# A routed two-mixture kernel: the second mixture's router logits from VectorE instead of TensorE, indices from VectorE, two result banks, scatter two steps behind, a packed schedule

## The chip, the cores and the metric

The kernel runs on one core of a Trainium2 chip. The metric is the device time of one execution in microseconds (us). The kernel before takes 753.04 us, the median of three runs (751.76 to 753.70).

## The reference

Attention over chunks of 64 tokens, then two mixtures of 8 experts (D = 512, F = 1024) over the same N = 2304 tokens; the second has a capacity of 576 tokens for an expert.

```python
x = attention_by_chunks(q, k, v)                  # 2304 x 512
# mixture 1 (w1, w2, w_gate, w_output_gate)
logits = x @ w_gate;  e = argmax(logits)
g = softmax(logits)[e] * sigmoid((x @ w_output_gate)[e])
x = g * (relu(x @ w1[e]) @ w2[e])
# mixture 2 (w1, w2, w_gate, capacity)
logits = x @ w_gate;  e = argmax(logits)          # these logits are what the change moves
g = softmax(logits)[e], 0 for tokens past an expert's capacity
out = g * (relu(x @ w1[e]) @ w2[e])
```

## The kernel before

**Stages.** Attention over 18 tiles of 128 tokens; routing 1; mixture 1 (in the code m = 0); routing 2; mixture 2 (m = 1). Routing sorts tokens by expert and pads each expert to whole tiles of 128: 20 tiles in either mixture. By the inputs, the tiles of experts 0 to 7 are 4, 1, 4, 3, 2, 1, 3, 2 in mixture 1 and 4, 4, 2, 5, 1, 2, 1, 1 in mixture 2.

**A tile.** POOL gathers 128 rows of x by an indirect DMA (`xg`). TensorE transposes them (L993), VectorE splits them in a high and a low part (`x_split`, L812 and L814), and TensorE forms the first product of 24 matmuls of 512 columns (three for each pair of chunk and half: high by high weights, low by high, high by low; L998 to L1000). VectorE applies relu (L804), TensorE transposes the hidden rows (L1020), VectorE splits them (`hidden_high` L821, `hidden_low` L827), and the second product, again 24 matmuls, goes to one PSUM bank. VectorE multiplies it by the gate (`scaled`, L842) into `y`, and POOL scatters `y` by an indirect DMA (L528). In mixture 1 the second mixture's router logits are formed beside it: TensorE transposes `y` (`result_T`, L1039), VectorE copies (`y_copy`, L835), TensorE multiplies by `wgate2` (`result_logits`, L1045), VectorE copies 8 columns behind the 512 of `y` (`logits_copy`, L846), and the scattered row has 520 columns.

**Order.** Each engine runs a written-out loop over tiles. `step(g)` on TensorE: transposes of h(g), first product of g+1, transposes of x(g+2), second product of g; in mixture 1 the transposes and the logits of y(g-1) lie inside the first product of g+1. `step(g)` on VectorE follows it, `scaled(g)` last. `scaled(g)` waits until scatter g-1 has landed, since there is one `y`, and the second product of g waits for `scaled(g-1)`, since there is one result bank.

**Weights.** An expert has 8 pieces of 512 KB (4 of w1, 4 of w2). SyncE loads a piece into one of 4 ring buffers, ScalarE rounds it to `wh` (L607), POOL subtracts to `wl` (`low_parts`, L423) and thereby frees the ring buffer. `wh` and `wl` hold two experts, so ScalarE waits for the last tile of the expert two before. A table made in routing (`pieces`, `middles`) tells POOL how many pieces to do in each of its steps. POOL's `step(g)`: read three entries of the table, pieces, scatter g-1, gather g+3, pieces. Before the scatter and before the gather POOL copies an index column (`sidx` L522, `gidx` L511) and waits for its own copy.

**Routing 2.** While VectorE works on the tables, POOL issues gather 0, does four pieces (the second half of expert 1's), and issues gather 1. `link` puts a wait between each VectorE instruction of the routing and the next.

Of the kernel before, what the change touches and what calls it, by code (L numbers as in the profile page):

```python
# [13 lines left out]
P = 128  # L14
# [9 lines left out]
def build(nc, q, k, v, wg1, wog1, w1a, w2a, wg2, w1b, w2b, cap, out):  # L24
# [31 lines left out]
    with ctx:  # L56
# [32 lines left out]
        wgate2 = sb("wgate2", [P, DC, E])  # L89
# [28 lines left out]
        scatter_at = [sb(f"scatter_at{m}", [P, NTAB], I32) for m in range(2)]  # L118
# [3 lines left out]
        pieces = [sb(f"pieces{m}", [P, NTAB], I32) for m in range(2)]  # L122

        middles = [sb(f"middles{m}", [P, NTAB], I32) for m in range(2)]
# [22 lines left out]
        at_pos = sb("at_pos", [P, 2, P, NH2], BF16)  # L147
        in_tile = sb("in_tile", [P, 2, NTAB, NH2], BF16)
        at_tile = sb("at_tile", [P, 2, NV, NTAB, NH2], BF16)
        at_gate = sb("at_gate", [P, 2, NG, NTAB, NH2], BF16)  # L150
        xg = sb("xg", [P, ROW])
        yT = sb("yT", [P, DC, P])
        h = sb("h", [P, F])
# [12 lines left out]
        hTh = sb("hTh", [P, FC, P], F32R)  # L166
        hTl = sb("hTl", [P, FC, P], F32R)
# [13 lines left out]
        ps_h, ps_hT, ps_y, ps_yT, ps_xT = b01, b23, b45[:, 0:BANK], b45[:, BANK:2 * BANK], b6  # L181
        ps_rank, ps_slot, ps_gate = b6, b7, b45

# [3 lines left out]
        s_w = sem("s_w")  # L187
        s_zero = sem("s_zero")
# [60 lines left out]
        yT_done = sem("yT_done")  # L249
        yT_here = sem("yT_here")  # L250
        yl_done = sem("yl_done")
        yl_here = sem("yl_here")
        si_here = [sem(f"si_here{m}") for m in range(2)]
# [5 lines left out]
        def at(x, g):  # L259

            return x[:, g:g + 1] if isinstance(g, int) else x[:, bass.ds(g, 1)]

# [132 lines left out]
        def _(pool):  # L395
# [35 lines left out]
            def due(m, g):  # L431


                lo = pool.value_load(at(pieces[m], g)[0:1, :], min_val=PX, max_val=2 * E * PX)
                hi = pool.value_load(at(pieces[m], g + 1)[0:1, :], min_val=PX, max_val=2 * E * PX)
                middle = pool.value_load(at(middles[m], g)[0:1, :], min_val=PX, max_val=2 * E * PX)
                return lo, middle, hi
# [14 lines left out]
            for m in range(2):  # L452
# [53 lines left out]
                def gather(g):  # L506

                    if reached(g, 1):
                        pool.wait_ge(g_in[m], g * 16)
                        pool.wait_ge(xT_done[m], g)  # L510
                    nc.gpsimd.tensor_copy(gidx[:, :], at(gather_at[m], g)).then_inc(gi_here[m], 1)  # L511
# [6 lines left out]
                def scatter(g):  # L518

                    if reached(g, 1):  # L520
                        pool.wait_ge(y_out[m], g * 16)
# [3 lines left out]
                    if m == 0:  # L525
                        pool.wait_ge(yl_here, g + 1)
# [5 lines left out]
                def step(g, ahead=True):  # L532
# [4 lines left out]
                    if reached(g, 1):  # L537
                        scatter(g - 1)
# [3 lines left out]

                step(0)
                with pool.Fori(1, total - 2) as g:
                    step(g)
                step(total - 2, ahead=False)
                step(total - 1, ahead=False)
                scatter(total - 1)
# [5 lines left out]
        def _(act):  # L554
            act.dma_start(wgate1[:, :, 0:E], wg1.rearrange("(c p) e -> p c e", p=P)).then_inc(s_w, 16)
            act.dma_start(wgate1[:, :, E:2 * E], wog1.rearrange("(c p) e -> p c e", p=P)).then_inc(s_w, 16)
            act.dma_start(wgate2[:, :, :], wg2.rearrange("(c p) e -> p c e", p=P)).then_inc(s_w, 16)
# [61 lines left out]
            act.wait_ge(routed, 1)  # L619
# [15 lines left out]
        def _(dve):  # L635
# [65 lines left out]
            for m in range(2):  # L701
# [129 lines left out]
                def y_copy(j):  # L831
                    dve.wait_ge(yT_done, j + 1)
                    if reached(j, 1):
                        dve.wait_ge(yl_done, j)
# [267 lines left out]
```

## Time and profile before

| what | us |
|---|---|
| median of three runs | 753.04 |
| the profiled execution's own time | 754.11 |
| its span, first to last instruction | 752.4 |
| mean granted TensorE clock (share of full) | 0.929 |
| TensorE busy | 642.0 (85%) |
| VectorE busy | 356.8 (47%) |
| POOL busy | 419.8 (56%) |
| ScalarE busy | 180.3 (24%) |

Attention takes the span to about 108 us, routing 1 to 124, mixture 1 to 430, routing 2 to 459, mixture 2 to the end. A group of the page gives the source line, the engine, the operation, the tiles that it writes and reads, the busy time and the idle time before it with what ended that. The rows that count stand in the section after the change.

### The profile page before, as it was taken

Reading aid. Unit: us, or ns where it says so; the run is one execution under the profiler, and the core shown is the slowest. Engines: PE = TensorE matmul, PEld = TensorE weight load, DVE = VectorE, ACT = ScalarE, POOL = GpSimd, SP = SyncE. Lnnn points to the kernel's source line nnn. Section 1 sums busy time; section 2 is a strip of 40 time slices with the busy share of each in tenths; the row PEclk is TensorE's granted clock in tenths of the full one; section 3 lists DMA queues with packets and bytes.
Section 4 is the critical chain, followed back from the end, with each engine's and each line's share of the span. In section 5 each row is a group of like instructions: output and inputs, shape, how many; then the busy total and the mean of one; then the engine's idle time right before and its main releaser. Section 6 shows DMA issues by size and latency. Waiting matters only on the chain.

```text
span 752.4 us, 15054 instructions
## 1 busy us (share of the span) xinstructions
PE 642.0 (85%) x4310; PEld 529.1 (70%) x4311; DVE 356.8 (47%) x652; ACT 180.3 (24%) x223; POOL 419.8 (56%) x351
## 2 busy tenths in 40 slices
PE   4898855999999999999987534999999999998653
PEld 3787844788887888877876423788888878886542
DVE  3887745454354354354334084545454364433240
ACT  2577631002420112422322200022023200243200
POOL 1046442256685657779778342116657763579760
PEclk9999985999999999999998655999999999999796
DMA  9999993043444425445554313114325532355500
GB/s 198 233 297 283 271 337 125 29 140 137 157 156 152 154 79 174 175 154 186 178 176 155 110 37 104 44 34 153 126 87 177 182 126 84 112 174 195 191 32 21
DMA packets 79690, 111.64 MB, mean 148 GB/s; under 512 B 28249, under 2 KB 46681, under 8 KB 79664
## 3 DMA queue, kind: packets, MB, share of 16 engines
q1 hardware_dynamic: 67616, 86.00, 37.0%
q0 software_dynamic: 8000, 25.17, 9.9%
q10 hardware_dynamic: 4048, 0.12, 0.3%
q8 instruction: 17, 0.28, 0.2%
q14 instruction: 9, 0.07, 0.0%
HBM read 92.48 MB, written 20.00 MB: 150 GB/s over the span
## 4 chain that ended last, share of the span: by engine, by line
PE 50%; POOL 14%; issue 12%; DVE 10%; POOLq 5%; DMA 5%; ACT 1%; ACTq 1%; DVEq 0%; SPq 0%
PE b L998 12%; PE b L999 12%; POOL wl L423 12%; PE b L1000 12%; PE b L925 2%; PE b L1020 2%; PE b L993 2%; PE b L903 2%; DVE owner L773 1%; DVE kT L665 1%; POOLq L423 1%; PE b L1045 1%; DVE xrow L676 1%; DMA x<-y,sidx 1%; PE b L913 1%
## 5 line engine op out<-in xcount | busy, mean ns | idle before, releaser
L423 POOL TENSOR_TENSOR wl<-ring,wh (+1 forms) x128 | 302.0, 2386 | 43.0 <-issue 21.3
L607 ACT CAST wh<-ring 128x1024 f32 (+1 forms) x112 | 112.8, 1047 | 479.2 <-PE b L1000 387.3
L998 PE MATMUL b<-wh,xTh 128*128 x320 | 135.0, 422 | 5.7 <-DVE xTl L814 3.7
L998 PE MATMUL b<-wh,hTh 128*128 x320 | 132.5, 414 | 7.5 <-DVE hTl L827 7.5
L842 DVE TENSOR_SCALAR y<-b,gates 128x512 f32<-128x512 f32 x40 | 30.0, 751 | 227.0 <-PE b L1000 103.2
L999 PE MATMUL b<-wh,xTl 128*128 x320 | 129.0, 403 | 0.0
L999 PE MATMUL b<-wh,hTl 128*128 x320 | 128.9, 403 | 0.0
L1000 PE MATMUL b<-wl,xTh 128*128 x320 | 128.0, 400 | 0.0
L1000 PE MATMUL b<-wl,hTh 128*128 x320 | 127.9, 400 | 0.0
L804 DVE TENSOR_SCALAR h<-b 128x512 f32<-128x512 f32 x80 | 54.8, 689 | 78.3 <-PE b L1000 78.1
L998 PEld LDWEIGHTS b<-wh,hTh 128*128 128x128 f32 x320 | 61.8, 193 | 21.3 <-issue 7.7
L998 PEld LDWEIGHTS b<-wh,xTh 128*128 128x128 f32 x320 | 61.6, 193 | 19.1 <-issue 7.2
L1000 PEld LDWEIGHTS b<-wl,hTh 128*128 128x128 f32 x320 | 61.3, 192 | 15.1
L1000 PEld LDWEIGHTS b<-wl,xTh 128*128 128x128 f32 x320 | 61.3, 192 | 14.8
L999 PEld LDWEIGHTS b<-wh,hTl 128*128 128x128 f32 x320 | 61.8, 193 | 12.8
L999 PEld LDWEIGHTS b<-wh,xTl 128*128 128x128 f32 x320 | 61.8, 193 | 11.4
L514 POOL DMA_INDIRECT xg<-x,gidx x36 | 37.8, 1049 | 31.4 <-POOL gidx L511 30.5
L827 DVE TENSOR_TENSOR hTl<-b,hTh 128x512 fp32r<-128x512 f32 x80 | 52.7, 680 | 0.0
L821 DVE CAST hTh<-b 128x512 fp32r<-128x512 f32 x80 | 51.1, 681 | 0.0
L993 PE MATMUL b<-ident,xg 128*128 128x128 f32 x168 | 26.8, 284 | 25.2 <-DMA xg<-x,gidx 12.2
L427 POOL DMA_DIRECT2D x<-xrow x18 | 10.2, 566 | 63.3 <-DVE xrow L676 63.3
L993 PEld LDWEIGHTS b<-ident,xg 128*128 128x128 f32 x168 | 21.5, 147 | 32.3 <-DMA xg<-x,gidx 13.5
(142 smaller groups left out, 663.1 us busy)
## 6 DMA issues: line engine op xcount, KB each, us to landing
ring<-in_moe_w SPq DMA_DIRECT2D x128, 512.0 KB, 3.2
vin<-in_v SPq DMA_DIRECT2D x72, 64.0 KB, 4.9
x<-xrow POOLq DMA_DIRECT2D x18, 256.0 KB, 6.1
out<-zeros SPq DMA_DIRECT2D x18, 256.0 KB, 3.8
qin<-in_q SPq DMA_DIRECT2D x6, 512.0 KB, 7.5
kin<-in_k SPq DMA_DIRECT2D x6, 512.0 KB, 6.9
qin<-in_q SPq DMA_DIRECT2D x2, 384.0 KB, 5.6
kin<-in_k SPq DMA_DIRECT2D x2, 384.0 KB, 5.9
```

The lines of the kernel that those rows point to most:

```text
L423: nc.gpsimd.tensor_tensor(low, src, high.bitcast(F32), ALU.subtract).then_inc(wl_here, 1)
L514: nc.gpsimd.indirect_dma_start(xg[:, 0:src.shape[1]], None, src, bass.IndirectOffsetOnAxis(ap=gidx[:, 0:1], axis=0), bounds_check=N - 1, o ...
L607: nc.scalar.copy(dst, ring[:, i % RING]).then_inc(wh_here, 1)
L804: nc.vector.tensor_scalar_max(h[:, cols], ps_h[:, cols], 0.0).then_inc((h0_here, h1_here)[half][m], 1)
L821: nc.vector.tensor_copy(hTh[:, chunks, :], ps_hT[:, half * BANK:(half + 1) * BANK].rearrange("p (c t) -> p c t", t=P)).then_inc((hTh0_here ...
L827: nc.vector.tensor_tensor(hTl[:, chunks, :], ps_hT[:, half * BANK:(half + 1) * BANK].rearrange("p (c t) -> p c t", t=P), hTh[:, chunks, :] ...
L842: nc.vector.tensor_scalar(y[:, 0:D], ps_y, at(gates[m], j), None, ALU.mult).then_inc(y_here[m], 1)
L903: last = nc.tensor.transpose(ps_aT[:, c * P:(c + 1) * P], xrow[:, (t - 1) % XS, c].rearrange("p e d -> p (e d)"), ident[:, :])
L993: last = nc.tensor.transpose(ps_xT[:, c * P:(c + 1) * P], xg[:, c * P:(c + 1) * P], ident[:, :])
L998: nc.tensor.matmul(dst, high, weights(wh, *wt), start=start, stop=False)
L999: nc.tensor.matmul(dst, low, weights(wh, *wt), start=False, stop=False)
L1000: return nc.tensor.matmul(dst, high, weights(wl, *wt), start=False, stop=stop)
```

## The change

- The logits of mixture 2: `wg2_rows` holds the router's 8 columns, each as a row of 512 on every partition (2 MB by one broadcast DMA on ScalarE's queue, behind routing 1). For every tile and expert VectorE issues one `scalar_tensor_tensor` of 128x512 (result x gate x row, with the sum as the accumulator's output): 8 a tile, of tile g-1 in step g, four behind relu(g+1, 0) and four behind `x_split(g+2)`. The transposes of y, both copies and the product with `wgate2` go.
- Two result banks take turns (`result_bank`); in mixture 1 `scaled(g-1)` stands at the end of step g, and the scatter is two steps behind.
- `gidx` and `sidx` are written by VectorE, out of PSUM copies of the tables (`next_rows`, and in `scaled`); POOL's two copies go.
- The schedule is one integer for a step, taken apart in registers, instead of three entries.
- The four pieces that POOL did inside routing 2 become part of mixture 2's schedule.
- The load of `wgate2` at the start goes.

```diff
@@ POOL
-                lo = pool.value_load(at(pieces[m], g)[0:1, :], ...)
-                hi = pool.value_load(at(pieces[m], g + 1)[0:1, :], ...)
-                middle = pool.value_load(at(middles[m], g)[0:1, :], ...)
+                cuts = pool.value_load(at(schedule[m], g)[0:1, :], min_val=0, max_val=2 ** 24 - 1)
+                lo, middle, hi = pool.snap(cuts % 256), pool.snap(cuts // 256 % 256), pool.snap(cuts // 65536)
...
                 if m == 1:
-                    for i in range((E + 1) * PX + PW, (E + 2) * PX):
-                        low_parts(i, i % RING)
                     pool.wait_ge(s_zero, 16 * NT)
...
-                    nc.gpsimd.tensor_copy(gidx[:, :], at(gather_at[m], g)).then_inc(gi_here[m], 1)
                     pool.wait_ge(gi_here[m], g - 2)
...
-                    nc.gpsimd.tensor_copy(sidx[:, :], at(scatter_at[m], g)).then_inc(si_here[m], 1)
-                    pool.wait_ge(si_here[m], g + 1)
-                    pool.wait_ge(y_here[m], g + 1)
+                    pool.wait_ge(y_here[m], g + 2)
...
-                        scatter(g - 1)
+                        scatter(g - behind)          # behind = (2, 1)[m]
@@ VectorE, routing
-                done = FIRST if m == 0 else (E + 2) * PX
+                done = FIRST if m == 0 else (E + 1) * PX + PW
...
+                # two more linked instructions pack pieces and middles into schedule[m],
+                # one more writes ps_gather; scatter_at becomes ps_scatter (PSUM)
@@ VectorE, mixtures
+                def next_rows(g):
+                    dve.wait_ge(xT_done[m], g)
+                    nc.vector.tensor_copy(gidx[:, :], at(ps_gather, g)).then_inc(gi_here[m], 1)
...
                 def scaled(j):
                     dve.wait_ge(y_done[m], j + 1)
                     if reached(j, 1):
                         dve.wait_ge(y_out[m], j * 16)
-                    nc.vector.tensor_scalar(y[:, 0:D], ps_y, at(gates[m], j), None, ALU.mult).then_inc(y_here[m], 1)
+                    nc.vector.tensor_copy(sidx[:, :], at(ps_scatter, j))
+                    if m == 0:
+                        dve.wait_ge(next_lg_here, (j + 1) * E)
+                        nc.vector.tensor_copy(y[:, D:ROW], next_lg)
+                    nc.vector.tensor_scalar(y[:, 0:D], result_bank(dve, j), at(gates[m], j), None,
+                                            ALU.mult).then_inc(y_here[m], 1)
+
+                def next_logits(j, experts):
+                    dve.wait_ge(y_done[m], j + 1)
+                    dve.wait_ge(y_here[m], j + 1)
+                    for e in experts:
+                        if e >= 2:
+                            dve.wait_ge(next_lg_here, j * E + e - 1)
+                        nc.vector.scalar_tensor_tensor(
+                            out=unread[:, e % 2], in0=result_bank(dve, j), scalar=at(gates[m], j), in1=wg2_rows[:, e, :],
+                            op0=ALU.mult, op1=ALU.mult, accum_out=next_lg[:, e:e + 1]).then_inc(next_lg_here, 1)
@@ TensorE
-                def result_T(j): ...          # 4 transposes of y
-                def result_logits(j): ...     # 4 products with wgate2
                 def second_product(g, first, before):
+                    dst = result_bank(pe, g)
```

VectorE's loop over the tiles of mixture 1, before (`hTh`, `hTl` are the hidden rows' parts, `xTh`, `xTl` those of x, b is any PSUM bank):

```order
L821 CAST hTh<-b 128x512 x2
L827 TENSOR_TENSOR hTl<-b,hTh 128x512
L834 REGISTER_ALU
L835 COPY yT<-b 128x512
L827 TENSOR_TENSOR hTl<-b,hTh 128x512
L800 REGISTER_ALU
L804 TENSOR_SCALAR h<-b 128x512
L846 COPY y<-b 128x8
L804 TENSOR_SCALAR h<-b 128x512
```

The same place now (`unread` is the product that nobody reads, `wg_rows` the router's rows):

```order
L837 CAST hTh<-b 128x512 x2
L843 TENSOR_TENSOR hTl<-b,hTh 128x512 x2
L811 REGISTER_ALU
L815 TENSOR_SCALAR h<-b 128x512
L866 ISA
L866 REGISTER_ALU
L866 SCALAR_TENSOR_TENSOR unread,b<-b,gates,wg_rows 128x512 x2
L865 ISA
L866 SCALAR_TENSOR_TENSOR unread,b<-b,gates,wg_rows 128x512
L865 REGISTER_ALU
L866 SCALAR_TENSOR_TENSOR unread,b<-b,gates,wg_rows 128x512
L815 TENSOR_SCALAR h<-b 128x512
```

The copy of the transposed y is gone and four multiply-and-sums stand between the two relus; four more stand at the end of the loop.

POOL in routing 2, before (`part` is the gate's last part of the routing):

```order
L481 TENSOR_TENSOR part<-rest,part 128x18
L488 DMA xg<-x,gather_at 128x520
L423 TENSOR_TENSOR wl<-ring,wh 128x1024 x4
L488 DMA xg<-x,gather_at 128x520
L270 TENSOR_LOAD ends
```

And now:

```order
L489 TENSOR_TENSOR part<-rest,part 128x18
L496 DMA xg<-x,gather_at 128x520 x2
L279 TENSOR_LOAD ends
L279 ISA x2
L496 DMA xg<-x,gather_at 128x520
```

The four pieces between gather 0 and gather 1 are gone from this place.

POOL's loop over the tiles of mixture 1, scatter and gather, before:

```order
L521 ISA
L522 ISA
L522 COPY sidx<-scatter_at 128x1
L528 DMA x<-y,sidx 2304x520
L509 ISA
L511 ISA
L511 COPY gidx<-gather_at 128x1
L514 DMA xg<-x,gidx 128x512
```

And now:

```order
L448 UNCONDITIONAL_BRANCH
L524 DMA x<-y,sidx 2304x520
L514 REGISTER_ALU
L516 DMA xg<-x,gidx 128x512
L448 REGISTER_ALU
```

Both copies are gone, and the two indirect DMAs stand one behind the other.

## Rows read from the trace of the kernel before

**Rows 1.** Page, part 4: the chain that ended last, by engine and line

```profile
PE b L998 12%; PE b L999 12%; POOL wl L423 12%; PE b L1000 12%; PE b L925 2%; PE b L1020 2%; PE b L993 2%; PE b L903 2%; DVE owner L773 1%; DVE kT L665 1%; POOLq L423 1%; PE b L1045 1%; DVE xrow L676 1%; DMA x<-y,sidx 1%; PE b L913 1%
```

**Rows 2.** Windows: one step of mixture 1 or 2 each; busy us (instructions)

```profile
core 0: us, PE busy (x) PEld busy (x) DVE busy (x) ACT busy (x) POOL busy (x), PEclk, DMA share, GB/s
136.03:149.82 13.79, 12.90 (x62) 10.24 (x61) 6.80 (x11) 0.00 (x0) 3.92 (x4) 1.00 0.11 39
163.67:177.51 13.84, 13.84 (x73) 11.52 (x72) 6.67 (x11) 3.89 (x4) 3.77 (x5) 1.00 0.11 39
497.14:509.65 12.51, 12.51 (x62) 10.23 (x60) 5.82 (x9) 3.89 (x4) 3.61 (x4) 1.00 0.13 42
```

**Rows 3.** Timeline of TensorE: steps 0 and 19 of either mixture start

```profile
136.03 0.60 PE L1020 MATMUL b<-ident,h 128*128 128x128 f32 x4
...
406.46 1.03 PE L1020 MATMUL b<-ident,h 128*128 128x128 f32 x8
...
470.83 1.17 PE L1020 MATMUL b<-ident,h 128*128 128x128 f32 x8
...
724.92 1.03 PE L1020 MATMUL b<-ident,h 128*128 128x128 f32 x8
```

**Rows 4.** Waits: us in total, times, longest

```profile
DVE y L842 <- DMA x<-y,sidx: 59.9, 10, 6.7
...
DVE iota_f L638 <- DMA cap_i<-in_capacity: 8.7, 1, 8.7
PE b L1039 <- DVE y L842: 9.6, 8, 2.7
```

**Rows 5.** Timeline of VectorE in mixture 1: start, us, what

```profile
207.09 0.75 DVE L842 TENSOR_SCALAR y<-b,gates 128x512 f32<-128x512 f32 x1 [5.70 <-DMA x<-y,sidx]
207.75 1.28 DVE L821 CAST hTh<-b 128x512 fp32r<-128x512 f32 x2
...
214.37 0.68 DVE L812 CAST xTh<-b 128x512 fp32r<-128x512 f32 x1
215.09 0.69 DVE L814 TENSOR_TENSOR xTl<-b,xTh 128x512 fp32r<-128x512 f32 x1
```

**Rows 6.** Timeline of VectorE: small and SBUF-to-SBUF instructions, attention and routing 2

```profile
9.71 0.17 DVE L642 CAST values<-token_i 128x36 bf16<-128x36 int32 x1
9.80 0.14 DVE L643 CAST cap_f<-cap_i 128x1 f32<-128x1 int32 x1
...
433.82 0.33 DVE L712 SCALAR_TENSOR_TENSOR order<-chosen,expert_no 128x144 f32<-128x144 f32 x1
...
437.65 0.31 DVE L735 TENSOR_TENSOR chosen<-chosen,over 128x144 f32<-128x144 f32 x1
```

**Rows 7.** Timeline of VectorE: the owner table in routing 1 and in routing 2

```profile
120.30 0.18 DVE L773 TENSOR_SCALAR owner<-owner_f 128x28 int32<-128x28 f32 x1
...
445.69 10.02 DVE L773 TENSOR_SCALAR owner<-owner_f 128x28 int32<-128x28 f32 x1
455.75 0.19 DVE L774 TENSOR_TENSOR soon<-owner_f 128x25 f32<-128x25 f32 x1
```

**Rows 8.** Timeline of POOL, routing 2 and the end of mixture 1

```profile
427.34 0.98 POOL L528 DMA_INDIRECT x<-y,sidx  x1 [4.77 <-DVE y L846]
...
446.42 9.24 POOL L423 TENSOR_TENSOR wl<-ring,wh 128x1024 fp32r<-128x1024 f32 x4
```

**Rows 9.** Timeline of POOL near the end of mixture 2

```profile
677.25 18.82 POOL L423 TENSOR_TENSOR wl<-ring,wh  x8
696.02 0.18 POOL L522 COPY sidx<-scatter_at 128x1 int32 x1
697.16 1.03 POOL L528 DMA_INDIRECT out<-y,sidx  x1 [0.96 <-POOL sidx L522]
698.19 0.20 POOL L511 COPY gidx<-gather_at 128x1 int32 x1
699.29 1.05 POOL L514 DMA_INDIRECT xg<-x,gidx  x1 [0.90 <-POOL gidx L511]
702.05 2.36 POOL L423 TENSOR_TENSOR wl<-ring,wh  x1 [1.72 <-issue]
```

**Rows 10.** Timeline, same stretch: TensorE, then VectorE's last waits

```profile
702.77 1.11 PE L993 MATMUL b<-ident,xg 128*128 128x128 f32 x4 [9.40 <-DMA xg<-x,gidx]
...
730.59 0.75 DVE L842 TENSOR_SCALAR y<-b,gates 128x512 f32<-128x512 f32 x1 [9.22 <-DMA out<-y,sidx]
```

More of the change, by code:

```diff
@@ L146, in build, with routed_by @@
             xrow = early("xrow", [P, XS, G, 2, DH])
[L147 to L150, printed above, removed]
+        with ExitStack() as routing:
+            def routed_by(name, shape):
+                return routing.enter_context(nc.sbuf_tensor(name, shape, BF16))
+            at_pos = routed_by("at_pos", [P, 2, P, NH2])
+            in_tile = routed_by("in_tile", [P, 2, NTAB, NH2])
+            at_tile = routed_by("at_tile", [P, 2, NV, NTAB, NH2])
+            at_gate = routed_by("at_gate", [P, 2, NG, NTAB, NH2])
+        hTh = sb("hTh", [P, FC, P], F32R)
+        hTl = sb("hTl", [P, FC, P], F32R)
+        h = sb("h", [P, F])
         xg = sb("xg", [P, ROW])
-        yT = sb("yT", [P, DC, P])
-        h = sb("h", [P, F])
         y = sb("y", [P, ROW])
@@ L165, in build @@
         xTl = sb("xTl", [P, DC, P], F32R)
[L166 to L167 removed]
+        unread = sb("unread", [P, 2, D])
+        wg2_rows = sb("wg2_rows", [P, E, D])
         b01 = bank("b01", 2)
@@ L541, in step @@
                     split(middle, hi)
+                behind = (2, 1)[m]
                 step(0)
-                with pool.Fori(1, total - 2) as g:
+                if m == 0:
+                    step(1)
+                    step(2)
+                with pool.Fori((3, 1)[m], total - 2) as g:
                     step(g)
@@ L547, in _ @@
                 step(total - 1, ahead=False)
+                if m == 0:
+                    scatter(total - 2)
                 scatter(total - 1)
@@ L619, in _ @@
             act.wait_ge(routed, 1)
+            for u in range(XS):
+                act.wait_ge(x_out[u], 16 * (NT // XS))
+            act.dma_start(wg2_rows[:, :, :].rearrange("p e d -> p (e d)"),
+                          wg2.rearrange("e d -> (e d)").unsqueeze(0).partition_broadcast(P)).then_inc(wg2_in, 16)
             with act.Fori(2, E) as e:
@@ L865, in step @@
                     if m == 0 and reached(g, 1):
-                        logits_copy(g - 1)
+                        next_logits(g - 1, range(0, E // 2))
                     if not tail:
                         relu(g + 1, 1)
+                        next_rows(g + 3)
                         x_split(g + 2)
-                    scaled(g)
+                    if m == 0 and reached(g, 1):
+                        next_logits(g - 1, range(E // 2, E))
+                        scaled(g - 1)
+                    if m == 0 and not reached(g, 1):
+                        dve.wait_ge(wg2_in, 16)
                     if m == 0 and tail:
-                        y_copy(g)
-                        logits_copy(g)
+                        next_logits(g, range(E))
+                    if m == 1 or tail:
+                        scaled(g)
                 expert_steps(dve, m, step)
@@ L1029, in second_product @@
                         for c in range(half * FC // 2, (half + 1) * FC // 2):
[L1030 removed]
+                            last = product(dst, hTh[:, c, :], hTl[:, c, :], (first, D * F // P // BANK + c),
                                            start=(c == 0), stop=(c == FC - 1))
                     last.then_inc(y_done[m], 1)
[L1034 to L1047 removed]
                 def step(g, head=False, tail=False):
```

97 lines of the change are left out of this document (30 added, 67 removed).

## The prediction

> **What bounds the kernel now.** I read the chain first [rows 1]: TensorE's product lines L998 to L1000 hold 36% of the span and POOL's low parts 12%, and a single VectorE instruction of the routing, L773, holds over 1%. So three places: TensorE inside the mixtures, POOL where experts are short, and one odd row. Then one step at a time, by windows [rows 2]: a step of mixture 1 takes 13.84 us with TensorE busy all of it, a step of mixture 2 takes 12.51 us, again full; VectorE is busy 6.67 and 5.82 us of them. The clock is full in both, so the difference, 1.33 us, is TensorE's work on the logits. Then the steps' starts [rows 3]: 19 steps of mixture 1 take 406.46 - 136.03 = 270.4 us. The first is 13.79 [rows 2]; with 18 at 13.84 that makes 262.9, so 7.5 us are stalls. Mixture 2: 254.1 us against 13.8 + 18 x 12.51 = 239.0, so 15.1 us are stalls. The waits name those of mixture 1 [rows 4]: 10 times `scaled` waits for a scatter, and 8 times (9.6 us) the transposes of y wait for `scaled`. Mixture 2 loses most at one place [rows 10]: TensorE idles 9.40 us for a gather that POOL issued late, behind eight pieces in a row [rows 9].
>
> **The change, part by part.** The sum is made against the profiled run's own 754.11 us; the median lies 1.07 lower.
>
> *Start.* VectorE's first instruction waits 8.7 us for the last of four small loads [rows 4], one of which goes. I count 0; the ends are 0 and -1, for the attention behind it is paced by its transfers.
>
> *Routing.* Three more small linked instructions in each, at about 0.2 us (0.19 for L774 [rows 7]): +0.6 each. In routing 2, L773 took 10.02 us and in routing 1, the same instruction, 0.18 [rows 7]. In routing 2 it ended (455.71) when POOL's four low parts did (446.42 + 9.24 = 455.66) [rows 8]: VectorE was shut out while POOL ran. The four pieces go from there, so L773 is short again: -9.8. All that follows on VectorE hangs on it, up to the `routed` that starts mixture 2. What is late next is gather 0, issued just before L773, about 3 us for its landing; the 14 linked instructions behind it, at some 0.2 us each, cover it. Net of the additions -9.2; if the indirect DMA of gather 0 holds it instead, 1 us less. The pieces come back in step 1 of mixture 2 as 9.4 us of POOL, which idles there; expert 1 starts at tile 4, so nothing waits for them.
> The Trainium skill (SBUF — State Buffer, "SBUF: two separate sides") says that VectorE in a two-port mode and GpSimd take one port pair in turn and the loser is blocked for the full instruction; the trace agrees, though here the block lasted four instructions, not one.
>
> *Mixture 1, TensorE.* 18 steps lose 1.33 us: -23.9, if nothing else becomes the limit. VectorE is the candidate. Its work in a step after, by distances from start to start: four halves of `hidden_high` and `hidden_low` at 0.60 (two take 1.28 with durations of 0.68 [rows 5]) = 2.4; two relus, same form, 1.2; `x_split` 0.72 (214.37 to 215.09) + 0.61 = 1.33; `scaled` 0.67 (207.09 to 207.75); three tiny copies at 0.09 to 0.18 (9.71 to 9.80 [rows 6]) and one wait for the last sum, 0.4 together. That is 6.0. To it come eight multiply-and-sums, of which no row shows one. From below: 0.60 is the distance of a plain PSUM instruction of that size. The pointer operand adds 0.07 (0.67 of `scaled`). The form itself adds nothing: at 128x144 it takes 0.33 against 0.31 for a `tensor_tensor` [rows 6]. The sum has to be written out; as a further small instruction that is 0.09 at the least, and if it waits until the pipeline is empty, 0.75 + 0.17 = 0.92 in all. From above: twice the length, about 1.2, see the rivals. I take 0.76, the row nearest (0.67 + 0.09): 8 x 0.76 = 6.1, the step 12.1 us. That is 0.4 under TensorE's 12.51: hidden, but barely. It is hidden up to 0.81 apiece; beyond, each 0.01 us costs 8 x 18 x 0.01 = 1.4 us. The ends: 0 and +16 (at 0.92).
> The Trainium skill (VectorE: DVE Perf Modes, "Two Vector instructions with no wait between them") says that an instruction with an accumulator output is two, the main one and an accumulator read. No row here shows one; it is in line with adding a second small instruction and gives no time for it.
> Order matters too: the four sums between the relus delay relu(g+1, 1) by 8.1 - 6.9 = about 1 us against its product, and x_split(g+2) with it, but TensorE needs them only in the next step, 4 us later. The second product of g waits for `scaled(g-2)`, because there are two banks: never late.
>
> *Mixture 1, stalls.* `scaled(g)` waited for scatter g-1 [rows 4]. Now it is done a step later and nothing on TensorE hangs on it for another; POOL also needs 2.2 us less for each tile (below). -7.5; the ends are 0 and -7.5.
>
> *Mixture 1, end.* Before, last step to last scatter: 427.34 - 406.46 = 20.9 us [rows 3, 8]. After: the hidden halves until 3.3 us after the step's start, eight sums of tile 18 to 9.4, `scaled(18)` to 10.5, eight of tile 19 to 16.6, copies and `scaled(19)` 1.2, POOL's start 0.4: 18.2. -2.7.
>
> *Mixture 2.* Same TensorE step. POOL's pair of scatter and gather loses 696.02 to 697.16 = 1.14 us and 698.19 to 699.29 = 1.10 us [rows 9], and the 1.72 us behind it, where three table entries are read, loses about 0.6 with one read. The chain to the late gather 19 (from the moment when ScalarE may round expert 5's w2, which is set by TensorE) holds one whole pair and the next one's two copies: 4.5 us less, so the stall of 9.4 becomes about 5. The two small stalls of the 15.1 (1.8 and 1.9 us) go nearly all: -3.4. At the end scatter 17, for which `scaled(18)` waits 9.22 us [rows 10], comes 2.2 us earlier against the step. Sum -10.1; the ends are -5 and -12. `gidx` on VectorE comes behind relu(g+1, 1), some 0.3 us later than the gather could start, and POOL's own 1.10 us for it is gone.
>
> *The broadcast load.* 2 MB behind routing 1, needed 25 us later, in a stretch with a DMA share of 0.11 [rows 2]: hidden.
>
> Sum: +0.6 - 9.2 - 23.9 - 7.5 - 2.7 - 10.1 = -52.8. As VectorE now has 0.4 us of slack in a step and any late step adds, I give 2 back: -50.8, so 703.3 in the profiled run, 702 to 703 as a median. I say 703.
>
> **The rivals.**
> *A. The sum costs a drained pipeline*, 0.86 to 0.95 apiece. VectorE bounds mixture 1 with 6.0 + 8 x 0.92 = 13.4 us a step, +16 us: 719. For it: VectorE's linked instructions never overlap, and I have no row. Against: the other PSUM instructions follow one another at 0.60 with durations of 0.68. Chance 0.20.
> *B. The stalls stay* (POOL is still late where experts are short, or VectorE's lateness meets it): half of the 7.5 + 10.1 comes back, and a few us more: 713. Chance 0.14.
> *C. Half speed.* 8 x 1.2 = 9.6, the step 15.6 us, 3.1 more than TensorE's, + 56 us: about 760, slower than before. The point from which it decides is 0.81 + 51 / 144 = 1.16 us apiece. Against it: the same form with two SBUF inputs, 0.33 us, would have taken 0.15 more at half speed [rows 6]. Chance 0.03.
> The Trainium skill (Vector Engine (DVE) Microarchitecture Reference, "Points that are easy to get wrong") states that this form with two SBUF sources that aren't bf16 halves its throughput, none of the ports being left for the accumulator. Here one source is PSUM; and for such an instruction without a sum rows 6 show no halving.
> *D. The port.* The sums read a row and a pointer from SBUF; if that shuts them out while POOL runs, as L773 was for 10.02 us [rows 7, 8], each block of four pieces (9.4 us) in mixture 1, 16 of them, stops VectorE for some 6 us: +90, about 790, slower. Against it: `hTl` reads PSUM and SBUF, `scaled` PSUM and a pointer, and neither is ever long. Chance 0.05.
>
> **How the numbers follow.** Forecast 0.58 (697 to 709), A 0.20, B 0.14, C 0.03, D 0.05. Low end: the bounds' gain, -1 and -2 and the 2 given back: 695, a little under it 693. High end: A with its 719 and some stall: 723. C and D lie outside. A measurement of this kernel tells 0.3%, 2.3 us, from no change. Faster: all but C and D, 0.92; same 0.01; slower 0.07.
>
> **What would show it.** L778 (the owner table) at 0.2 to 1.2 us in routing 2. In mixture 1 steps of 12.51 us with VectorE busy over 12; the sums' rows 0.67 to 0.85 us from start to start. TensorE's transposes of h in a regular beat with no gap. In mixture 2 one idle of about 5 us where 9.40 was. I am wrong if the steps of mixture 1 are longer than 12.6 us, with TensorE waiting for `hTl` or `h`, or if sums are stretched beside L432.

## The result, and the profile after

The changed kernel takes 709.05 us (median of 4 runs, 705.91 to 711.15) against 753.37 (4 runs, 751.76 to 755.91): a ratio of 0.9405 [0.936, 0.9451], 44 us less. Its profiled execution took 710.0 us with a span of 708.3 and a mean granted clock of 0.931; the one of before had 752.4 and 0.929. So 44.1 us in the spans stand against the 50.8 forecast: the direction and the mechanism of the steps held, and the gain was 7 us smaller. The median, 709.05, lies at the upper edge of the band that the forecast gave itself (697 to 709).

First the page's part 1 and the start of its chain by line, then two groups of its part 5, and behind them the first of the two as it was before (line, engine, operation, out<-in, count, busy us, mean ns, idle before):

```profile
PE 613.4 (87%) x4070; PEld 503.5 (71%) x4071; DVE 448.4 (63%) x1036; ACT 180.2 (25%) x223; POOL 406.8 (57%) x275
...
PE b L1024 20%; PE b L1026 19%; PE b L1025 19%; PE b L1046 4%; PE b L1019 2%; DMA ring<-in_moe_w 2%; PE b L951 2%; POOL wl L432 2%; PE b L929 2%; DVE kT L670 2%; ACT wh L608 1%; DVE xrow L681 1%; DVE qT L668 1%; PE b L939 1%; DMA x<-y,sidx 1%
...
L1024 PE MATMUL b<-wh,hTh 128*128 x320 | 132.8, 415 | 10.8 <-DVE hTl L843 10.8
...
L866 DVE SCALAR_TENSOR_TENSOR unread<-b,gates,wg_rows 128x512 f32<-128x512 f32 x160 | 110.1, 745 | 1.2 <-PE b L1026 1.2
...
L998 PE MATMUL b<-wh,hTh 128*128 x320 | 132.5, 414 | 7.5 <-DVE hTl L827 7.5
```

TensorE's product lines now hold 58% of the chain where they held 36% [rows 1], POOL's low parts 2% instead of 12%, and the row `owner` is gone from it. VectorE took 110 us more of sums and TensorE hardly noticed: its product holds the chain. TensorE waits 10.8 us at L1024 for `hTl`, in three places (5.70, 1.07 and 4.02 us); before it was 7.5 in one place, at the end of mixture 2. The 5.70 and the 1.07 are new, and no term of the forecast has them.

The table divides the span at the first instruction of routing 1 and at TensorE's transposes of h (L1020 before, L1046 after), as rows 3 did. They follow for after.

```profile
137.53 1.17 PE L1046 MATMUL b<-ident,h 128*128 128x128 f32 x8
...
376.86 1.03 PE L1046 MATMUL b<-ident,h 128*128 128x128 f32 x8
...
433.60 1.17 PE L1046 MATMUL b<-ident,h 128*128 128x128 f32 x8
...
684.31 1.03 PE L1046 MATMUL b<-ident,h 128*128 128x128 f32 x8
```

| stretch | before | after | change | forecast |
|---|---|---|---|---|
| start to routing 1 | 108.35 | 110.35 | +2.0 | 0 |
| routing 1 to step 0 of mixture 1 | 27.68 | 27.18 | -0.5 | +0.6 |
| 19 steps of mixture 1 | 270.43 | 239.33 | -31.1 | -31.4 |
| last step to last scatter | 20.88 | 22.64 | +1.8 | -2.7 |
| last scatter to step 0 of mixture 2 | 43.49 | 34.10 | -9.4 | -9.2 |
| 19 steps of mixture 2 | 254.09 | 250.71 | -3.4 | -7.9 |
| last step to the end | 27.48 | 23.99 | -3.5 | -2.2 |

The first row can't be told from the spread between executions: over the thirteen profiled executions after, with the same attention in each, routing 1 started between 107.05 and 114.14 us. Below, "without attention" is the span less that start: 644.05 before, 597.95 after.

**A step of mixture 1.** Windows of one step (columns as in rows 2):

```profile
237.86:250.40 12.54, 12.54 (x62) 10.23 (x61) 12.51 (x32) 0.00 (x0) 11.31 (x6) 1.00 0.48 151
```

TensorE has the 12.5 us and the 62 matmuls of a step of mixture 2 [rows 2]. VectorE reads full as well, which doesn't mean that it bounds: it does 32 instructions here and 29 in the next step, where it is busy 11.07 us of 12.52. Its timeline (start, us, what):

```profile
249.29 0.74 DVE L866 SCALAR_TENSOR_TENSOR unread<-b,gates,wg_rows 128x512 f32<-128x512 f32 x1
249.96 0.14 DVE L866 DVE_READ_ACCUMULATOR unread<-b,gates,wg_rows 128x1 f32 x1
249.96 0.75 DVE L866 SCALAR_TENSOR_TENSOR unread<-b,gates,wg_rows 128x512 f32<-128x512 f32 x1
250.63 0.14 DVE L866 DVE_READ_ACCUMULATOR unread<-b,gates,wg_rows 128x1 f32 x1
...
254.38 1.28 DVE L837 CAST hTh<-b 128x512 fp32r<-128x512 f32 x2
...
265.67 1.28 DVE L837 CAST hTh<-b 128x512 fp32r<-128x512 f32 x2
```

From one sum to the next 0.67 us: the reading of the accumulator is a row of 0.14 us that begins with the next sum and costs nothing. From 254.38 to 265.67, a step without a wait, VectorE needs 11.29 us, 1.2 under TensorE.

**Routing 2.** The owner table, 10.02 us before [rows 7]:

```profile
417.84 0.18 DVE L778 TENSOR_SCALAR owner<-owner_f 128x28 int32<-128x28 f32 x1
```

**The end of mixture 1.** VectorE, TensorE and POOL behind the last step's start (376.86):

```profile
380.39 0.16 DVE L852 CAST sidx<-b 128x1 int32 x1 [1.88 <-DMA x<-y,sidx]
...
381.24 1.28 DVE L837 CAST hTh<-b 128x512 fp32r<-128x512 f32 x2
382.44 1.28 DVE L843 TENSOR_TENSOR hTl<-b,hTh 128x512 fp32r<-128x512 f32 x2
...
390.11 0.16 DVE L852 CAST sidx<-b 128x1 int32 x1 [0.97 <-DMA x<-y,sidx]
...
392.26 0.75 DVE L866 SCALAR_TENSOR_TENSOR unread<-b,gates,wg_rows 128x512 f32<-128x512 f32 x1 [1.21 <-PE b L1026]
```

```profile
383.60 0.79 PE L1024 MATMUL b<-wh,hTh 128*128 x1 [5.70 <-DVE hTl L843]
384.18 0.63 PE L1025 MATMUL b<-wh,hTl 128*128 x1
384.61 0.63 PE L1026 MATMUL b<-wl,hTh 128*128 x1
...
399.50 0.98 POOL L524 DMA_INDIRECT x<-y,sidx  x1 [6.60 <-DVE y L856]
```

Read downward: `scaled(17)`, of which `sidx` is the first instruction, waits for a scatter's landing; the hidden halves stand behind it in VectorE's order; TensorE idles 5.70 us for them, and its matmuls then follow one another at 0.43 us until 388.9 and at 0.23 behind it. The window of that product; its granted clock is a mean of the two levels (0.50 of full is 1.2 GHz, 1.00 is 2.4):

```profile
383.60:392.20 8.60, 8.41 (x24) 6.37 (x24) 6.47 (x20) 0.15 (x1) 3.70 (x4) 0.67 0.45 162
```

The kernel before had the same wait at the same place, and its trace showed it before the forecast was made:

```profile
409.31 0.75 DVE L842 TENSOR_SCALAR y<-b,gates 128x512 f32<-128x512 f32 x1 [6.68 <-DMA x<-y,sidx]
```

That is 2.9 us behind the start of the last step (406.46), and its hidden halves ended 6.6 us behind it, at 413.05. TensorE waited there too, 2.70 us before the transposes of y.

**The late gather of mixture 2.** POOL, TensorE and VectorE, the stretch of [rows 9, 10]:

```profile
636.58 18.89 POOL L432 TENSOR_TENSOR wl<-ring,wh  x8
655.64 1.02 POOL L524 DMA_INDIRECT out<-y,sidx  x1 [0.17 <-issue]
656.96 1.03 POOL L516 DMA_INDIRECT xg<-x,gidx  x1 [0.30 <-issue]
658.01 9.31 POOL L432 TENSOR_TENSOR wl<-ring,wh  x4
667.49 1.01 POOL L524 DMA_INDIRECT out<-y,sidx  x1 [0.16 <-issue]
```

```profile
661.35 1.11 PE L1019 MATMUL b<-ident,xg 128*128 128x128 f32 x4 [6.88 <-DMA xg<-x,gidx]
663.53 0.79 PE L1024 MATMUL b<-wh,hTh 128*128 x1 [1.07 <-DVE hTl L843]
...
660.29 0.16 DVE L852 CAST sidx<-b 128x1 int32 x1 [15.92 <-DMA out<-y,sidx]
```

The pair of scatter and gather costs POOL 1.32 us from start to start (2.13 in rows 9), and the idle fell from 9.40 to 6.88. But the scatter issued at 655.64 stood behind the same eight pieces, and `scaled(16)` waited 15.92 us for it. `hTl` came late through it, by 1.07 us more. The windows of the second product behind it, before and after:

```profile
703.54:710.61 7.07, 7.07 (x27) 5.60 (x25) 2.39 (x4) 0.00 (x0) 7.07 (x4) 0.79 0.53 160
663.53:671.77 8.24, 8.24 (x25) 6.48 (x26) 2.67 (x6) 0.00 (x0) 5.82 (x4) 0.66 0.72 240
```

So the shorter idle bought nothing here: the gather's rows arrive 2.5 us sooner behind the step's start, the product starts 1.1 sooner, it takes 1.2 longer at a lower granted clock, and the step is 23.94 us where it was 23.87. The 3.4 us that the 19 steps gained are the two small stalls (14.42 and 14.31 us before, 12.53 and 12.54 now).

**The landings.** POOL's indirect DMAs, median us from issue to landing, before and then after:

```profile
xg<-x,gidx POOLq DMA_INDIRECT x36, 3.4
x<-y,sidx POOLq DMA_INDIRECT x20, 3.1
...
xg<-x,gidx POOLq DMA_INDIRECT x36, 3.8
x<-y,sidx POOLq DMA_INDIRECT x20, 4.3
```

The forecast left these as they were, and they became longer. The late gather was issued 3.4 us sooner behind its step's start and took 4.3 us instead of 3.4 to land; the scatter just ahead of it took 4.5 instead of 3.0. With POOL's copies put back (below) the gathers take 3.4 again. Why they became longer isn't shown. Two things changed at once: scatter and gather are issued 1.3 us apart and not 2.1, and the scatter 0.17 us behind the last piece and not 1.1; and in the run with the scatter one step behind, mixture 1 has 1.3 us between them and a median of 3.4 for the scatter, so the distance alone doesn't do it.

### The profile page after: what moved, and what is told of

Its sections match the earlier page's. It is cut to its first block, busy times and chain, and to the rows that moved or that the text cites. A ratio compares the mean times of both kernels' runs of the same rounds, so it can differ in the third digit from the quotient of the medians.

```text
span 708.3 us, 14771 instructions
## 1 busy us (share of the span) xinstructions
PE 613.4 (87%) x4070; PEld 503.5 (71%) x4071; DVE 448.4 (63%) x1036; ACT 180.2 (25%) x223; POOL 406.8 (57%) x275
## 4 chain that ended last, share of the span: by engine, by line
PE 72%; DVE 11%; DMA 6%; issue 4%; POOL 2%; ACT 2%; POOLq 1%; ACTq 0%; DVEq 0%; SPq 0%
PE b L1024 20%; PE b L1026 19%; PE b L1025 19%; PE b L1046 4%; PE b L1019 2%; DMA ring<-in_moe_w 2%; PE b L951 2%; POOL wl L432 2%; PE b L929 2%; DVE kT L670 2%; ACT wh L608 1%; DVE xrow L681 1%; DVE qT L668 1%; PE b L939 1%; DMA x<-y,sidx 1%
## 5 line engine op out<-in xcount | busy, mean ns | idle before, releaser
L1024 PE MATMUL b<-wh,hTh 128*128 x320 | 132.8, 415 | 10.8 <-DVE hTl L843 10.8
L1024 PE MATMUL b<-wh,xTh 128*128 x320 | 131.8, 412 | 5.5 <-DVE xTl L830 3.7
L866 DVE SCALAR_TENSOR_TENSOR unread<-b,gates,wg_rows 128x512 f32<-128x512 f32 x160 | 110.1, 745 | 1.2 <-PE b L1026 1.2
L852 DVE CAST sidx<-b 128x1 int32 (+1 forms) x40 | 6.6, 164 | 130.3 <-PE b L1026 67.4
L1024 PEld LDWEIGHTS b<-wh,hTh 128*128 128x128 f32 x320 | 61.9, 193 | 25.1 <-issue 11.7
L1024 PEld LDWEIGHTS b<-wh,xTh 128*128 128x128 f32 x320 | 61.1, 191 | 19.7 <-issue 6.7
L1025 PEld LDWEIGHTS b<-wh,hTl 128*128 128x128 f32 x320 | 61.9, 193 | 13.3
L843 DVE TENSOR_TENSOR hTl<-b,hTh 128x512 fp32r<-128x512 f32 x80 | 51.2, 681 | 0.0
L524 POOL DMA_INDIRECT out<-y,sidx x20 | 20.3, 1014 | 45.5 <-DVE y L856 43.6
```

The source lines that it names most:

```text
L524: nc.gpsimd.indirect_dma_start(dst, bass.IndirectOffsetOnAxis(ap=sidx[:, 0:1], axis=0), y[:, 0:width], None, bounds_check=N - 1, oob_is_er ...
L843: nc.vector.tensor_tensor(hTl[:, chunks, :], ps_hT[:, half * BANK:(half + 1) * BANK].rearrange("p (c t) -> p c t", t=P), hTh[:, chunks, :] ...
L866: nc.vector.scalar_tensor_tensor(out=unread[:, e % 2], in0=result_bank(dve, j), scalar=at(gates[m], j), in1=wg2_rows[:, e, :], op0=ALU.mul ...
L1024: nc.tensor.matmul(dst, high, weights(wh, *wt), start=start, stop=False)
L1025: nc.tensor.matmul(dst, low, weights(wh, *wt), start=False, stop=False)
```

## The experiments

Each run is told against the kernel before on its own chip. The unchanged repetition is the zero of the first four.

**The changed kernel again**

> The changed kernel once more, to stand beside the others of this chip. Both theories: the ratio to the kernel before is 0.935 to 0.945, the steps of mixture 1 are 12.5 us, L778 of routing 2 takes 0.2 us.

709.24 us (6 runs), ratio 0.9404 [0.9366, 0.9442]. Without attention 597.04. The result repeats.

**The pieces back in routing 2**

```diff
+                    for i in range((E + 1) * PX + PW, (E + 2) * PX):
+                        low_parts(i, i % RING)
                     pool.wait_ge(s_zero, 16 * NT)
-    done = FIRST if m == 0 else (E + 1) * PX + PW
+    done = FIRST if m == 0 else (E + 2) * PX
```

> The four low parts of expert 1 stand between gather 0 and gather 1 of routing 2 again, all else is as in the changed kernel. My theory: VectorE is shut out of its owner table (L778) while POOL runs, 10.0 us where it was 0.2, and mixture 2 starts 9.8 us later: +9 to +10 us. Rival (the long instruction came from something else that the change took, such as the copies of the indices or the transposes): L778 stays under 1.5 us and the time moves by less than 2.

718.62 us, ratio 0.9505 [0.9469, 0.9542], 9.4 more than the repetition by the medians; from the last scatter to step 0 of mixture 2 it takes 44.23 us and not 34.10. VectorE and POOL in routing 2:

```profile
421.23 10.02 DVE L780 TENSOR_SCALAR owner<-owner_f 128x28 int32<-128x28 f32 x1
```

```profile
421.96 9.24 POOL L432 TENSOR_TENSOR wl<-ring,wh 128x1024 fp32r<-128x1024 f32 x4
```

The same 10.02 us as in rows 7, ending (431.24) when the fourth piece does (431.20). This edit alone is worth what its term says, and the block lasted, here as before, to the end of POOL's four back-to-back instructions.

**The small load back at the start**

```diff
+        wgate2 = sb("wgate2", [P, DC, E])
...
+            act.dma_start(wgate2[:, :, :], ...).then_inc(s_w, 16)   # before cap_i's
```

> A third small load of 16 KB (not used) stands before the capacity's on ScalarE's queue again, and VectorE and TensorE wait for it. Theory: the start gained 1 us by its absence and the transfers of the attention took it back, so with it VectorE starts 0.7 to 1.0 us later and the time is the same within 1 us. Rival (its absence shifted the transfers against each other and cost the 2 us by which the attention ended later): routing 1 starts 2 us earlier, at 108.3, total -1 to -2 us.

VectorE and TensorE wait for it as well. 709.96 us, ratio 0.9409 [0.9371, 0.9447]; VectorE's first instruction starts at 8.65 us and not at 7.95, and routing 1 at 110.41, as in the changed kernel (110.35). No difference: the start's term is 0.

**Two y**

The last five tiles of either mixture take turns between two `y` and two `sidx`; for this the 20 tiles are constants and those steps are written out, and there POOL issues a scatter only when the one before it has landed.

```diff
-        y = sb("y", [P, ROW])
-        sidx = sb("sidx", [P, 1], I32)
+        y = sb("y", [P, 2, ROW])
+        sidx = sb("sidx", [P, 2], I32)
...
-                        dve.wait_ge(y_out[m], j * 16)
+                        dve.wait_ge(y_out[m], landed_before(j) * 16)   # j - 1 from tile 15 on
```

> Two buffers for y and for its index in the last five tiles of either mixture (the kernel takes the number of tiles, 20, as a constant there and writes these steps out), so that scaled(j) waits for scatter j-2 and not for scatter j-1. My theory: what was missing from the forecast lies in late scatters, which hold scaled and behind it the low half of the hidden rows that the second product waits for: in mixture 1 last step to last scatter falls from 22.6 to 20 us or less, in mixture 2 step 17 from 23.9 to about 21 us and the end by 2 to 3 more, together -5 to -8 us. Rival (POOL's rate of pieces and gather 19 hold the end of mixture 2, the half clock the end of mixture 1): step 17 stays at 23 or more, total within 2 us of the changed kernel.

699.40 us (693.36 to 701.50), ratio 0.925 [0.9208, 0.9292], 9.8 less than the repetition. TensorE before the last second product of mixture 1, then of mixture 2:

```profile
380.95 0.50 PE L1045 MATMUL b<-wh,hTh 128*128 x1 [2.13 <-DVE hTl L858]
...
679.38 0.49 PE L1045 MATMUL b<-wh,hTh 128*128 x1 [2.25 <-DVE hTl L858]
```

2.13 us idle instead of 5.70. From the last step to the last scatter it takes 17.95 us, not 22.64, which is what I had forecast (18.2) for the kernel with one `y`; the step with the late gather takes 21.55, not 23.94, and the end 21.91, not 23.99. The other steps came out shorter too, 12.39 us in place of 12.53, which no theory had said.

**A spare tile, nothing else** (that last point by itself; nobody uses the 2080 bytes for each partition)

```diff
         y = sb("y", [P, ROW])
+        spare = sb("spare", [P, ROW])
```

> The changed kernel with an unused SBUF tensor of 2080 bytes behind y, so that the tensors behind it (xTh and xTl among them) lie at the addresses that they have in the run with two buffers for y, whose steps were 12.39 us and not 12.53. Theory: the addresses do it; steps of 12.39, 38 x 0.13 = -5 us. Rival (the written-out VectorE and POOL steps or the second buffer did it): 12.53 and no change.

Steps of 12.39 us again: 19 of them 237.79 in mixture 1 and 247.51 in mixture 2, against 239.33 and 250.71. The total is 707.18 us, ratio 0.932 [0.9269, 0.9371]; without attention 593.4, some 4 less than the changed kernel's. By the total alone, 2 us under the repetition's, this wouldn't be clear of noise; the steps show it. The groups of part 5 say which matmuls it is, in the changed kernel and then with the spare tile:

```profile
L1025 PE MATMUL b<-wh,hTl 128*128 x320 | 128.9, 403 | 0.0
L1025 PE MATMUL b<-wh,xTl 128*128 x320 | 127.8, 400 | 0.0
...
L1026 PE MATMUL b<-wh,hTl 128*128 x320 | 128.7, 402 | 0.0
L1026 PE MATMUL b<-wh,xTl 128*128 x320 | 125.8, 393 | 0.0
```

Only the first product became faster, whose operands xTh and xTl are allocated behind `y` and so moved with the spare tile: its matmuls follow one another at 0.228 us instead of 0.233, and 24 of them make the 0.13 us of a step. The second product's operands hTh and hTl, allocated ahead of `y`, stayed where they were and so did its 0.233. So of the 12 us that two `y` gain without attention (597.95 to 585.8), 4 to 5 are where the buffers lie and 7 to 8 the waits. Why an address matters isn't settled.

**One, and three, sums more for each tile**

```diff
-                        next_logits(g, range(E))
+                        next_logits(g, range(E + 3))          # or E + 1; likewise range(E // 2, E + 3)
```

> One further multiply-and-sum for each tile of mixture 1 (nine). Theory: VectorE's step 12.0 us stays under TensorE's 12.53, so the steps stay at 12.5 and only the two last tiles cost 0.67 each: +1 to +2 us. Rival (lateness counts before VectorE is full): steps of 12.7 and more, +4 or more.

> Three further multiply-and-sums for each tile of mixture 1 (eleven; their results go to spare columns and are not used). Theory: VectorE's step is 11.3 us in the changed kernel, each sum 0.67 with nothing for the accumulator's read, TensorE's step 12.53; with three more VectorE needs 13.3 and sets the step: 18 x 0.8 = 14 us and 4 more at the end, +16 to +20. Rival (a VectorE that is late harms TensorE long before it is full, since relu and the halves of x come later): more than +25. Other rival (the two banks hide it): +4.

One more: 710.12 us, ratio 0.9422 [0.9391, 0.9453], steps still 12.5. Three more: 721.62 us, ratio 0.9564 [0.9536, 0.9591]. Two neighbouring steps of that run:

```profile
238.64 1.03 PE L1046 MATMUL b<-ident,h 128*128 128x128 f32 x8
...
251.95 1.03 PE L1046 MATMUL b<-ident,h 128*128 128x128 f32 x8
```

13.3 us, which is 11.29 + 3 x 0.67. The steps stay at 12.5 until VectorE's lead is used up, in the sixth (12.67), so the price was 12 us and not 16 to 20. The two runs measure a sum at 0.67 us and the slack between one and two of them.

**POOL copies its indices again**

```diff
                 def gather(g):
...
+                    nc.gpsimd.tensor_copy(gidx[:, :], at(gather_at[m], g)).then_inc(gi_here[m], 1)
...
                 def scatter(g):
...
+                    nc.gpsimd.tensor_copy(sidx[:, :], at(scatter_at[m], g)).then_inc(si_here[m], 1)
+                    pool.wait_ge(si_here[m], g + 1)
```

> POOL copies both index columns itself again and waits for its copies, as in the kernel before; the rest is the changed kernel. Theory: 2.2 us more of POOL for each tile; hidden in the steps of mixture 1 and 2 behind TensorE (two banks), seen where POOL is the limit: step 17 of mixture 2 from 23.9 to 25.5 or more and the ends of both mixtures, +3 to +6 us. Rival (most of the gain on the stalls of mixture 1 was this and not the two banks): steps of 14 us come back in mixture 1, +8 or more.

Ahead of its copies POOL waits again for the landing of the scatter and of the gather that used the column before, and for the transposes of those rows; in the rows below none of these waits costs anything. 729.16 us, ratio 0.9657 [0.9627, 0.9687]: 20 more, mixture 1 by 14.4 of them (19 steps 253.68; seven of them 13.0 to 16.6 us where they had been 12.5). My 3 to 6 fell, the rival's 8 or more held. POOL in a stretch with four pieces a step:

```profile
275.06 0.19 POOL L530 COPY sidx<-scatter_at 128x1 int32 x1
276.19 1.04 POOL L534 DMA_INDIRECT x<-y,sidx  x1 [0.93 <-POOL sidx L530]
278.32 1.05 POOL L522 DMA_INDIRECT xg<-x,gidx  x1 [0.90 <-POOL gidx L519]
280.10 9.45 POOL L434 TENSOR_TENSOR wl<-ring,wh  x4 [0.73 <-issue]
289.50 0.18 POOL L530 COPY sidx<-scatter_at 128x1 int32 x1
```

A round takes POOL 289.50 - 275.06 = 14.44 us. With its indices from VectorE the changed kernel's round takes 12.01 in the same mixture (scatters at 350.61 and 362.62 with four pieces between) and 667.49 - 655.64 = 11.85 in mixture 2. TensorE's step, 12.53, lies between. So where four pieces are due in every step for several steps, POOL bounds with its copies and doesn't without them.

**The scatter one step behind in mixture 1**

```diff
-                behind = (2, 1)[m]
+                behind = 1
```

> In mixture 1 POOL scatters g-1 in step g, one step behind and not two, before gather g+3; the rest is the changed kernel. Theory: the scatter must wait for scaled(g-1) at the end of VectorE's step, and the gather and the pieces queue behind it on POOL, which is idle for some 8 us a step: stalls wherever pieces are due, +8 to +25 us in mixture 1. Rival (POOL has time to spare; the two steps buy only the wait): under +3.

708.72 us, ratio 0.935 [0.9301, 0.9399]; without attention 596.6 against 597.95 and 597.04 with two, so no difference that can be told. The 19 steps took 2.4 us more (241.73), and the end of mixture 1 gave more than that back: 18.0 us from the last step to the last scatter in place of 22.64. My 8 to 25 fell, the rival held: this part of the change buys nothing by itself. TensorE before the last second product of mixture 1:

```profile
383.82 0.49 PE L1019 MATMUL b<-wh,hTh 128*128 x1 [2.06 <-DVE hTl L838]
```

Here `scaled(17)`, at 379.39, found scatter 16 long landed (it was issued at 368.33; in the changed kernel at 375.61, behind four pieces). So this run and the one with two `y` cure the end of mixture 1 by two different edits, and both reach the 18 us of the forecast: what lengthened it was the wait of `scaled` for a scatter that the change had put a step later.

**One result bank in mixture 1**

```diff
-                        pe.wait_ge(y_here[m], g)
+                        pe.wait_ge(y_here[m], g + 1 if m == 0 else g)    # result_bank: always the first
```

> Mixture 1 uses one result bank; the second product of g therefore waits for scaled(g-1), which stands at the end of VectorE's step. Theory: it starts 12.3 us into the step and not 7.2, the step becomes about 18 us, + 90 to 105 us. Rival (VectorE catches up, since it has 1.2 us of slack and the sums could be early): step under 15 us, under +45.

871.90 us, ratio 1.1569 [1.1533, 1.1605], 163 more where I expected 90 to 105. TensorE before one second product, then the window of that step:

```profile
310.86 0.79 PE L1026 MATMUL b<-wh,hTh 128*128 x1 [6.06 <-issue]
```

```profile
297.71:318.15 20.44, 14.38 (x61) 11.46 (x60) 11.44 (x28) 0.00 (x0) 2.86 (x3) 0.83 0.21 66
```

The second product starts behind the step's sums, 13.2 us into the step where 12.3 was expected, and it takes 7.3 us and not 5.6, the granted clock of the step being 0.83 with 6 us of idle in it. In four of the steps more is lost on top. With the sums on VectorE the second bank is needed.

**Dummy transposes**, with the spare tile: 7 before the first rows of either mixture, 6 behind them, 24 behind the last hidden transposes.

```diff
+                for i in range(7):
+                    nc.tensor.transpose(b23[:, 0:P], ident[:, :], ident[:, :])
                 pe.wait_ge(routed, m + 1)
...
+                    if tail:
+                        for i in range(24):
+                            nc.tensor.transpose(b01[:, 0:P], ident[:, :], ident[:, :])
```

> The spare tensor, and unused transposes on TensorE where it waits: 7 before a mixture's first rows, 6 behind them, 24 behind the last tile's transposes, so that it is not idle before the first and the last products. Theory (the clock falls to 1.2 GHz in these waits and the products that follow pay for it): beside the spare tensor's effect 2 to 2.5 us less at each head and 2.5 to 3 at each end, -9 to -11, so 694 to 697 us. Rival (the heads and the ends are set by VectorE and POOL): no gain beyond the spare tensor's, or a loss of 1 to 2 where the transposes stand in the way.

703.11 us, ratio 0.929 [0.9241, 0.9338], not the 694 to 697 expected; without attention 591.95 against 593.4 with the spare tile alone. The heads are no shorter. At the end of mixture 1 the last product started 3 us after the transposes instead of 5.5 with none, and the last scatter came no earlier (22.05 and 21.92 us behind the step), since `scaled` waited for a scatter's landing there. Only the very end gained (22.48 us against 25.39 with the spare tile and 23.99 in the changed kernel). The half clock is a cost, but behind the wait for a scatter it is mostly covered.

**Two y and the head transposes**

> Two buffers for y in the last five tiles of either mixture (tile count 20 taken as a constant), and the unused transposes at the two heads. Theory: 699.4 less 2 x 2 to 2.5 us: about 695. Rival: 699 to 701.

694.90 us (693.45 to 702.26), ratio 0.9205 [0.9138, 0.9273]; without attention 584.65 against 585.8 with two `y` alone. Of the 4 to 5 us expected of the heads at most 1 came. It has the lowest median of all, though its interval overlaps that of two `y` alone, and it beats both kernels, at the price of a number of tiles that is fixed.

## Why the prediction was right, and where it fell short

- *Start, routing 1*: 0 as forecast; -1.1 beside the forecast between routing 1 and the first step: the first product of mixture 1 took 7.62 us and not 8.80, at a mean granted clock of 0.78 and not 0.66, which nothing in the forecast foresaw. That is luck; the +2.0 of attention lies within the spread between executions.
- *Mixture 1, TensorE and stalls*: -31.1 for -31.4. Every one of the 19 steps took 12.51 to 12.56 us except for the first (13.78, as before). TensorE's part of it is read from the windows (73 matmuls a step before, 62 now); no run puts the logits alone back on TensorE. The attribution of the stalls was wrong in part. I gave them to the scatter's extra step and mentioned POOL's 2.2 us a tile beside it. The runs showed that those 2.2 us carry them (with the copies back +14.4 in mixture 1), and that the step more behind saves only 2.4 in the steps, which the end of the mixture loses again.
- *The size of a sum*: 0.76 forecast, 0.67 measured. I had added a row for the accumulator's read; it overlaps. So rival A (0.92 apiece) fell, and C and D with it: the 160 sums take 745 ns on the mean, beside POOL's pieces too.
- *Routing 2*: -9.4 for -9.2, and undone alone it costs 9.4.
- *Mixture 1, end*: +1.8 for -2.7, a mis-sized term by 4.5 us. The step that failed reads "the hidden halves until 3.3 us after the step's start". They ended at 383.7, 6.8 us after it. It was taken from an undisturbed step, though the trace of before had 6.6 us at this very place. The term then goes: 18.2, +3.5 for the halves, -1.4 for 16 sums at 0.67, +1.0 for the second wait for a scatter, +1.2 for TensorE's product at half clock, makes 22.5 (22.64 measured). The last 1.2 belongs to this execution: in the repetition, with 22.1, VectorE waits only 0.3 us there. I had written that nothing on TensorE hangs on the scatter "for another" step. It does where POOL has just done four pieces and the order puts `scaled` ahead of the hidden halves: that scatter (375.61) landed 4.6 us behind its issue, where the median before was 3.1.
- *Mixture 2*: -6.9 for -10.1 (steps and end), off by 3.2. The two small stalls went (-3.7 for -3.4), and the end gained more than forecast (-3.5 for -2.2). The mis-sized term is the large stall: -4.5 forecast, +0.1 measured. Its idle was to fall from 9.40 to about 5 and fell to 6.88, since the gather was issued 3.4 us sooner and not 4.5, and landed 0.9 later. I had also priced it by its idle alone, though the step had lost 23.87 - 12.51 = 11.4 us: the product at a lower clock was a cost that stood in the trace and got nothing. And I followed the gather and let the other chain through the same eight pieces stand: scatter, its landing, `scaled`, `hTl`, second product. Two `y` break that chain, and with them this step and both ends take 2.4, 4.7 and 2.1 us less, of which the addresses explain little. That the chain costs this much was shown by that run; how it divides into idle, landings and half clock was only read from the rows.
- *2 us given back for lateness*: not needed in the steps (1.2 us of slack).
- *Rival B*: its 713 is nearer to the profiled run's 710.0 than my 703.3 is. Its mechanism, POOL late where experts are short, is what happened in the step of the late gather and at the end of mixture 1; the stalls inside mixture 1, which it also expected back, went whole.
- *The range*: its low end doesn't add up. 703 less 1, 2 and 2 is 698, and not 695. The measured time lies on the other side.

The deviations add up: -52.8 + 2.0 (attention) - 1.1 (routing 1) + 0.3 (mixture 1) + 4.5 (its end) - 0.2 (routing 2) + 3.2 (mixture 2) = -44.1, the measured difference of the spans.

## What to carry to other kernels

Work may be moved to an engine that has room in a step, but look at the order in which that engine stands: a wait of its last instruction for a DMA's landing is paid by all that stands behind it, and it shows at the ends, where nothing else covers it. When several chains run through one late stretch, shorten all of them or count the longest that stays. To know whether a helper engine bounds, add up its whole round in the worst stretch (here 14.44 or 12.01 us) and set it against the step (12.53). Price a stall by what its step lost, and not by the idle row alone. And look up in the trace of before the very place that a term is about, not a typical one.

## What the runs showed of the hardware

- A multiply-and-sum with an accumulator output leaves two rows, the second (0.14 us) at the same start as the next instruction; from start to start 0.67 us for 128x512 with one PSUM source and one in SBUF, 0.07 above a plain PSUM instruction [rows 5].
- TensorE's step is 12.53 or 12.39 us by where buffers lie in SBUF: one unused tile does it. Only the matmuls whose x operand changed its place became faster, 0.228 us apart and not 0.233; why isn't shown.
- An indirect scatter of 128 rows landed 2.6 to 4.6 us behind its issue in the changed kernel; its median in mixture 1 was 3.1 us before and 4.3 after.
- Behind idles of 5.70 and 6.88 us TensorE's matmuls came 0.43 us apart (granted clock 0.50, 1.2 GHz) and the second product took 8.6 and 8.2 us instead of 5.6. The length of the idle alone doesn't tell it: in the kernel before, behind 9.40 us, it took 7.1, and with two `y`, the product behind 2.13 us went at 0.23 throughout, and the one behind 2.25 us fell to 0.43 after its first two matmuls.
- VectorE's small int32 write was shut out for 10.02 us in two kernels, both times to the end of four back-to-back POOL instructions, while the 160 sums with one SBUF source were never stretched (739 to 751 ns).
The Trainium skill (SBUF — State Buffer, "SBUF: two separate sides") speaks of the loser being blocked for the full instruction; in both kernels with the pieces in routing 2 it was blocked for the whole row of four instructions. The Trainium skill (Vector Engine (DVE) Microarchitecture Reference, "Points that are easy to get wrong") states that the sum's form with two SBUF sources that aren't bf16 halves its throughput; with one source in PSUM, as here, the trace shows 745 ns for 512 columns, no halving, and no run here has a sum with two.
